# Attention of the next block beside a matmul stream: another order of its steps, of their loads, and of the sums for the second matmul

## What is computed

```python
scores = scale * np.matmul(q_c, k_full.transpose(0, 1, 3, 2))
scores = scores - np.max(scores, axis=-1, keepdims=True)
a = np.exp(scores)
a = a / (np.sum(a, axis=-1, keepdims=True) + 1e-09)
out[:, :, c_start:c_end] = np.matmul(a, v_full)
...
h = x @ w_in            # 3072 x 512 by 512 x 2048
g = h * np.cos(h)
x = g @ w_out           # by 2048 x 512
...
h = np.maximum(np.maximum(x @ w1, x @ w2), x @ w3)   # by 512 x 768 each
return h @ w_out        # by 768 x 512
```

## Time and profile before

| | |
|---|---|
| median of 3 runs | 1004.28 us (1001.45 to 1005.49) |
| the profiled execution's own time | 1003.52 us |
| its span in the trace | 1001.7 us |
| TensorE matmul busy | 962.1 us (96%) |
| VectorE / ScalarE / GpSimd busy | 675.9 (67%) / 516.0 (52%) / 210.2 us (21%) |
| mean granted TensorE clock | 0.983 |

### The profile page before, as it was taken

One profiled execution on the slowest core, in us unless ns is written; L12 is line 12 of the kernel. 1 busy time (PEld: TensorE's weight loads), 2 busy tenths in 40 slices (PEclk: granted clock), 3 DMA queues, 4 the chain that ended last, 5 costly groups with the idle time before them and its releaser, 6 DMA issues.

```text
span 1001.7 us, 18402 instructions
## 1 busy us (share of the span) xinstructions
PE 962.1 (96%) x7564; PEld 933.3 (93%) x7564; DVE 675.9 (67%) x926; ACT 516.0 (52%) x689; POOL 210.2 (21%) x231
## 2 busy tenths in 40 slices
PE   5989999999999999999999999999999999999998
PEld 4878889898989899989999999999999999999998
DVE  4355666566665568997998989866736546577761
ACT  1586786867778788333433334543323224444441
POOL 3341111112121212100100000662100000584610
PEclk6799999999999999999999999999999999999999
DMA  9983656574653434443445434432020031324532
GB/s 223 227 212 101 185 149 187 145 201 129 192 165 111 149 131 155 149 145 125 149 145 172 148 106 133 140 120 92 32 95 32 33 127 48 121 95 146 192 116 84
DMA packets 65395, 135.41 MB, mean 135 GB/s; under 512 B 5920, under 2 KB 27424, under 8 KB 65312
## 3 DMA queue, kind: packets, MB, share of 16 engines
q1 hardware_dynamic: 54944, 98.58, 34.2%
q0 software_dynamic: 10368, 35.66, 10.8%
HBM read 87.03 MB, written 47.19 MB: 134 GB/s over the span
## 4 chain that ended last, share of the span: by engine, by line
PE 73%; ACT 10%; DVE 9%; DMA 4%; issue 3%; POOL 1%; SPq 1%; DVEq 0%; ACTq 0%
PE ps L595 23%; PE ps L597 22%; PE ps L596 22%; PE ps L611 2%; DVE work L1178 2%; ACT work L901 2%; PE ps L636 2%; DVE units L1215 2%; ACT work L896 1%; ACT work L903 1%; PE ps L645 1%; DMA early_qk<-qk_in 1%; DVE ssum L1145 1%; ACT work L893 1%; ACT work L872 1%
## 5 line engine op out<-in xcount | busy, mean ns | idle before, releaser
L595 PE MATMUL ps<-units 128*128 128x384 f32 (+1 forms) x1940 | 611.1, 315 | 8.3 <-DVE units L1215 2.0
L597 PE MATMUL ps<-units 128*128 128x384 f32 (+1 forms) x1940 | 602.9, 311 | 0.0
L596 PE MATMUL ps<-units 128*128 128x384 f32 (+1 forms) x1940 | 602.6, 311 | 0.0
L595 PEld LDWEIGHTS ps<-units 128*128 128x128 f32 x1940 | 369.4, 190 | 20.2 <-issue 6.9
L596 PEld LDWEIGHTS ps<-units 128*128 128x128 f32 x1940 | 369.6, 191 | 0.0
L597 PEld LDWEIGHTS ps<-units 128*128 128x128 f32 x1940 | 369.2, 190 | 0.0
L921 ACT CAST units<-work 128x1024 fp32r<-128x1024 f32 x96 | 85.7, 939 | 123.9 <-DVE work L1201 106.6
L1076 ACT COPY work<-ps 128x384 f32<-128x384 f32 (+1 forms) x144 | 63.6, 454 | 146.9 <-PE ps L597 146.8
L1173 DVE SCALAR_TENSOR_TENSOR work<-work 128x768 f32<-128x768 f32 x64 | 62.2, 972 | 71.8 <-ACT work L896 71.8
L1215 DVE TENSOR_TENSOR units<-work,units 128x1024 fp32r<-128x1024 f32 x96 | 102.1, 1105 | 12.2 <-ACT units L921 12.2
L486 POOL DMA_DIRECT2D g_dram<-work x64 | 46.8, 731 | 291.4 <-DVE work L1178 286.7
(11 more groups left out here) (96 smaller groups left out, 845.4 us busy)
## 6 DMA issues: line engine op xcount, KB each, us to landing
g_dram<-work POOLq DMA_DIRECT2D x64, 384.0 KB, 3.3
work<-g_dram SPq DMA_DIRECT2D x48, 512.0 KB, 3.7
work<-qk_in SPq DMA_DIRECT2D x36, 384.0 KB, 5.3
work<-v_in SPq DMA_DIRECT2D x40, 256.0 KB, 5.0
work<-w_in POOLq DMA_DIRECT2D x40, 256.0 KB, 3.6
h_dram<-work SPq DMA_DIRECT2D x24, 384.0 KB, 2.9
work<-h_dram SPq DMA_DIRECT2D x18, 512.0 KB, 3.9
work<-y_dram SPq DMA_DIRECT2D x8, 768.0 KB, 6.5
```

Of the source, the lines that this page charges most:

```text
L595: pe.matmul(o, wh, mh, start=start, stop=False, skip_group_check=onto)
L596: pe.matmul(o, wh, ml, start=False, stop=False, skip_group_check=onto)
L597: return pe.matmul(o, wl, mh, start=False, stop=stop, skip_group_check=onto)
```

## The change

- **Opening:** on TensorE the second `turn_probs` now comes ahead of the third `scores_of`; raw w_in is loaded behind all values of block 0, and its casts (`high_wi(0)` to `(3)`) come behind the last `x_high`.
- **Block 0** (`attend0`): the scores of subs 3 to 5 move from beside f = 0, 2, 4 to f = 2, 5, 8, the exponentials from f = 5 to f = 9, the transposes of the probabilities to f = 10, 11, 12, the values to f = 12, 13, 14, the transposes of the output to f = 13, 14, 15. The scores of subs 6 to 8, which stood here, move to block 1.
- **Block 1** (`attend1`): has what block 0 had before, the scores of its own three subs among it, and those of block 2 at f = 8, 11, 14.
- **Blocks 2 to 6** (`attend`): the first `turn_out` moves from f = 4 to f = 5; `values(n + 1)` comes right ahead of `scores_of` at f = 6 (was f = 7), `values(n + 2)` likewise at f = 9 (was 11); the last `turn_out` at f = 11. VectorE's `x_low(n)` moves from f = 4 to f = 6, behind a `normalise` and a `shift`.
- **Loads:** values have three buffers for three blocks in place of two, and SyncE's list alternates values and scores' operands in the new order; g's first load comes before the last values.
- **Weight and g sums:** `sums_w1(5)` and `sums_g(0)` are made in block 6, the other g sums of block 7 come earlier, `sums_w1(6)` moves from f = 14 to f = 10, `sums_w1(7)` from the unit stage (behind unit 2) to f = 14 of block 7, with a buffer of its own; `low_w1(6)` and `low_w1(7)` stand together ahead of `sums_g(3)`. `load_w1(6)` stays where it was; `load_w1(7)` is issued right behind it, once it has landed.
- **y stage:** two more buffers let `y_sum(blk, 2)` and `(blk, 3)` be made ahead, before the block begins; they lie in the buffer of `load_v2(0)`, which therefore waits for the end of y's last block load (`y_ready` = 28) and not for `w2_ready` = 9 as before.

```diff
+        def y_extra(blk, i):
+            at = 9984 + 768 * (i - 3)
+            return work[:, at:at + 768].rearrange("p (k t) -> p k t", k=2) if blk and i > 2 else raw_y[:, 4, :, :]
+
+        def source_y(blk, p):
+            if p in (5, 6, 4):
+                return y_extra(blk, {5: 2, 6: 3, 4: 4}[p])
+            return raw_y[:, {1: 0, 7: 1, 2: 2, 3: 3}[p], :, :]
...
@@ -327,8 +338,9 @@
                     sp.wait_ge(g_stored[i % 3], 16 * (i // 3) + 16)
                 if n >= 2:
                     sp.wait_ge(g_ready, n - 1)
+                elif n == 1:
+                    sp.wait_ge(pv_done, SUBS)
                 else:
-                    sp.wait_ge(pv_done, SUBS)
                     sp.wait_ge(qk_done, SUBS)
...
@@ -393,30 +405,41 @@
             load_qk(0)
             load_qk(1)
             load_v(0)
-            load_wi(0)
             load_qk(2)
             load_v(1)
             load_v(2)
-            for f in range(1, 6):
+            for f in range(4):
                 load_wi(f)
             for n in range(NSUB, 2 * NSUB):
                 load_qk(n)
-                load_wi(2 * n)
-                load_wi(2 * n + 1)
+                load_wi(2 * n - 2)
+                load_wi(2 * n - 1)
             for n in range(NSUB, 2 * NSUB):
                 load_v(n)
-                if n < 2 * NSUB - 1:
-                    load_wi(2 * n + 6)
-                    load_wi(2 * n + 7)
+                load_wi(2 * n + 4)
+                load_wi(2 * n + 5)
             for n in range(2 * NSUB, 3 * NSUB):
                 load_qk(n)
-            load_v(2 * NSUB)
+                load_v(n)
             load_qk(3 * NSUB)
-            for n in range(2 * NSUB + 1, SUBS):
-                load_v(n)
+            load_qk(3 * NSUB + 1)
+            load_v(3 * NSUB)
+            load_qk(3 * NSUB + 2)
+            load_qk(3 * NSUB + 3)
+            for n in range(3 * NSUB, SUBS, NSUB):
+                if n + 3 == SUBS:
+                    load_g(0)
+                load_v(n + 1)
+                load_v(n + 2)
                 if n + 3 < SUBS:
-                    load_qk(n + 3)
-            for n in range(4):
+                    if n + 4 < SUBS:
+                        load_qk(n + 4)
+                    load_v(n + 3)
+                    if n + 5 < SUBS:
+                        load_qk(n + 5)
+                    if n + 6 < SUBS:
+                        load_qk(n + 6)
+            for n in range(1, 4):
...
             def load_w1(p):
-                if p:
+                if p == FPAIRS - 1:
+                    pool.wait_ge(o_ready, SUBS)
+                elif p:
...
             def load_v2(v):
-                if v == 0:
-                    pool.wait_ge(w2_ready, UNITS)
-                else:
-                    pool.wait_ge(y_ready, 7 * NBLK2)
+                pool.wait_ge(y_ready, 7 * NBLK2)
...
@@ -561,7 +583,8 @@
                     load_w1(5)
                 if t == 7 and p == 3:
                     load_w1(6)
-            load_w1(7)
+                    pool.wait_ge(w1_landed, 32 * 7)
+                    load_w1(7)
             load_w2(0)
...
-            def attend_first(f):
+            def attend0(f):
                 n = NSUB
+                if f == 2:
+                    scores_of(n)
+                elif f == 5:
+                    scores_of(n + 1)
+                elif f == 8:
+                    scores_of(n + 2)
+                elif f == 10:
+                    turn_probs(n)
+                elif f == 11:
+                    turn_probs(n + 1)
+                elif f == 12:
+                    turn_probs(n + 2)
+                    values(n)
+                elif f == 13:
+                    turn_out(n)
+                    values(n + 1)
+                elif f == 14:
+                    turn_out(n + 1)
+                    values(n + 2)
+                elif f == 15:
+                    turn_out(n + 2)
...
                     turn_probs(n + 1)
+                elif f == 5:
                     turn_out(n)
                 elif f == 6:
                     turn_probs(n + 2)
+                    values(n + 1)
                     if later:
                         scores_of(n + NSUB)
-                elif f == 7:
-                    values(n + 1)
                 elif f == 8:
                     turn_out(n + 1)
-                elif f == 9 and later:
-                    scores_of(n + NSUB + 1)
+                elif f == 9:
+                    values(n + 2)
+                    if later:
+                        scores_of(n + NSUB + 1)
                 elif f == 11:
-                    values(n + 2)
-                elif f == 12:
                     turn_out(n + 2)
-                    if later:
-                        scores_of(n + NSUB + 2)
+                elif f == 12 and later:
+                    scores_of(n + NSUB + 2)
 
...
+            def beside0(f, i):
+                n = NSUB
+                if f + 4 < NF:
+                    high_wi(f + 4)
+                if f == 9:
+                    exps(0, NSUB, n + NSUB)
+                elif f == 11:
+                    copy_probs(n)
+                elif f == 15:
+                    x_high(n + 2)
+                if f % 2:
+                    evacuate(i)
+                    if f == 11:
+                        copy_probs(n + 1)
+                    elif f == 13:
+                        x_high(n)
+                    if i:
+                        cosine(i - 1)
+                if f == 12:
+                    copy_probs(n + 2)
+                elif f == 14:
+                    x_high(n + 1)
...
+            def beside_last(f, i):
+                if f % 2:
+                    evacuate(i)
+                    cosine(i - 1)
+                if f == 1:
+                    high_w1(5)
+                elif f == 4:
+                    high_g(0, 0)
+                    high_g(0, 1)
+                elif f == 8:
+                    high_g(1, 0)
+                    high_g(1, 1)
+                elif f == 12:
+                    high_g(2, 0)
+                    high_g(2, 1)
+
...
-                if i == 2:
-                    dve.wait_ge(y_ready, 7 * blk + 2)
-                if i == 3:
-                    dve.wait_ge(y_ready, 7 * blk + 4)
-                o, in0, in1 = ((e, b12, b11), (b12, b22, b12), (e, b22, e), (e, b21, e))[i]
+                b11, b12, b21, b22 = [raw_y[:, q, :, :] for q in range(4)]
+                e = [y_extra(blk, j) for j in (2, 3, 4)]
+                if not blk and i >= 2:
+                    dve.wait_ge(y_ready, 2 * i - 2)
+                elif blk and i == 2:
...
+            def beside(t, f, i):
+                n = NSUB * (t + 1)
+                if f == 3:
+                    normalise(n)
+                elif f == 9:
+                    normalise(n + 2)
+                if f % 2:
+                    pair(i)
+                if f == 2:
+                    sums(0, NSUB, NSUB + t + 1)
+                elif f == 5:
+                    sums_w1(t - 1)
+                elif f == 6:
+                    normalise(n + 1)
+                    if t < NBLK - 2:
+                        shift(n + NSUB)
...
+            def beside_last(f, i):
+                if f % 2:
+                    pair(i)
+                if f == 0:
+                    sums_g(1)
+                elif f == 2:
+                    low_w1(5)
+                elif f == 4:
+                    low_g(0, 0)
+                    low_g(0, 1)
+                elif f == 6:
+                    sums_g(2)
+                elif f == 8:
+                    low_g(1, 0)
+                    low_g(1, 1)
+                elif f == 10:
+                    sums_w1(6)
+                elif f == 12:
+                    low_g(2, 0)
+                    low_g(2, 1)
+                elif f == 14:
+                    sums_w1(7)
+
...
                     y_low(blk + 1, 5)
-                    y_sum(blk + 1, 2)
+                    y_low(blk + 1, 2)
                 if n < UNITS_ALL:
                     c12(n)
                 if n and before < UNITS_A and before % NB2:
                     c21(before)
                 if renew:
-                    y_low(blk + 1, 2)
                     y_low(blk + 1, 6)
                     y_low(blk + 1, 3)
                 if renewed:
                     y_low(blk, 7)
-                    y_sum(blk, 3)
                     y_low(blk, 4)
+                if n < UNITS_A and u == UNITS - 2 and blk < NBLK2 - 1:
+                    y_sum(blk + 1, 2)
+                    y_sum(blk + 1, 3)
                 if n < UNITS_A and u == UNITS - 3 and blk < NBLK2 - 1:
                     y_sum(blk + 1, 0)
                     y_sum(blk + 1, 1)
```

317 lines of the change are left out of this document (159 added, 158 removed).

## The result

The changed kernel takes 1018.63 us (median of 4 runs, 1014.81 to 1024.56), the kernel before 1004.88: a ratio of 1.0147, 95% interval 1.0115 to 1.0179. It is slower by some 14 us. 5 were forecast, and the time lies outside the stated range. The profiled execution has a span of 1015.5 us, against 1001.7.

The account below looks back on a forecast made before the run. TensorE's matmuls, busy 96% of the span, were taken to bound the kernel. Terms +5.8 + 0 - 7.3 + 4.0 + 2.5 = +5.0 on the profiled 1003.5 gave 1008.5 us, range 995 to 1015.

Parts of the forecast that it names:

- Blocks 2 to 6, -7.3 forecast: Blocks 2 to 6: five 1.59 us waits of the first turn_out for normalise go; -7.3, bounds -7.9 and -4.8.
- counted from the durations it ends 0.6 ahead of the second `turn_out`: Blocks 2 to 6: x_low(n), in its new place behind normalise(n + 1) and a shift, is still 0.6 us early.
- Block 0: Block 0: evacuate(3) waits for tile 0's store, 9.0 us to land, delaying exponentials and x_low; block 1 starts at 90.3, +5.8.
- Rival 2: Block 0: tile 0's store lands as fast as the median one, 5.0 us less, 1003.5; chance 0.15.
- The opening: Start of the kernel: block 0 begins some 0.8 us earlier, at 32.0, counted inside block 0's sum.
- Block 1: Block 1: takes over block 0's old work; first turn_out waits 2.4 us against 2.6 before; 0, bounds -1.5 and +2.
- Unit stage: +4.0 forecast: Block 7 and unit stage: TensorE's waits total 8 us against 4.0 before; +4.0, bounds -4.0 and +6.
- VectorE's stand: Block 7: VectorE stands still 6.0 us ahead of sums_w1(6), waiting for its load behind a store on GpSimd.
- still cost: Unit stage: the results' sums at the border of the first eight units cost 1.3 us as before.
- y stage: +2.5 forecast: y stage: load_v2(0) waits for y_ready = 28, three v2 sets follow one another; +2.5, bounds 0 and +5.5.
- The rival for the case "slower": y stage: v2 sets cost 5.5 not 2.5 us, plus 1.5 for half clocks in block 0; 1013, chance 0.15.
- new waits in blocks 2 to 6 for `x_low`: Blocks 2 to 6: a listed sign that the prediction is wrong; no size given.

Follow-up runs that it names:

- e3_w1load: Changed kernel with load_w1(1) to load_w1(5) issued behind the store of tile 8t + 5, not 8t + 6, on GpSimd: 1005.88 us, ratio 1.0007.
- a1_xlow: Changed kernel with VectorE's x_low(n) ahead of normalise(n + 1) and the shift in blocks 2 to 6, weight sums behind them: 1006.8 us, ratio 1.0029.
- a3_xlow_qk: Changed kernel with both the edits of a1_xlow and a2_qk: 1002.3 us, ratio 0.9995 to the kernel before.
- a2_qk: Changed kernel with SyncE loading the scores' operands of sub n + 5 ahead of the values of sub n + 3: 1018.13 us, ratio 1.0148.
- e1_w17_old: d2_all with weight set 7 as in the kernel before (load behind last store, sums_w1(7) at unit 2, low_w1(7) at unit 4): 992.55 us, ratio 0.9868.
- e2_w17_mid: d2_all keeping the early load of set 7, but sums_w1(7) ahead of unit 2's g sums and low_w1(7) ahead of unit 3's: 992.5 us, ratio 0.9874.
- b1_yback: Changed kernel with the y stage as before: no buffers for sums ahead, load_v2(0) behind w2_ready = 9: 1015.63 us, ratio 1.0116.
- e4_mid_w1load: e2_w17_mid with the edit of e3_w1load: 992.11 us, ratio 0.987 to the kernel before.
- d2_all: d1_block0_old with b1_yback's edit, sums_w1(6) back at f = 14, load_w1(7) behind tile 61's store, sums_w1(7) behind the last gated: 992.92 us, ratio 0.9889.
- d1_block0_old: a3_xlow_qk with blocks 0 and 1 in the order of before but the changed opening: 995.13 us, ratio 0.9889.

## Why the prediction was wrong

- **Blocks 2 to 6, -7.3 forecast, +8.3 measured. The step that failed** is "counted from the durations it ends 0.6 ahead of the second `turn_out`". It ended 1.8 to 2.5 us behind. The durations were right; the start of the chain was not. The count took `evacuate` to come with TensorE's step, as it does in the trace of before (197.28 and 197.42). But it is held there by a landing store, which came just then, and the landing does not get earlier with TensorE. In block 3 of the changed kernel `evacuate` is 2.5 us behind the step; without this `x_low` would have ended some 0.7 ahead of the second `turn_out` (an estimate: 2.5 less the wait of 1.83). e3_w1load shows the cause, a1_xlow and a3_xlow_qk that the list could have absorbed it. A second omission: the order of SyncE's list, where a load of values stands ahead of the third scores' load (4.3 us of waits). By a2_qk that is worth little alone, and by a3_xlow_qk against a1_xlow 3 to 5 us (1006.8 to 1002.3, by the ratios 3.4) once the other is mended. A third is the granted clock, 0.96 in blocks 5 and 6, which the term put at nothing. The prediction's bound of -4.8 allowed 0.5 us for each late `x_low`, a quarter of what came.
- **The gain itself was right**: with the list and the loads mended, blocks 2 to 6 give 7.0.
- **Block 0: right in its chain.** The store of tile 0 was issued at 46.27, and the evacuate that waited for it began 9.5 us later (9.0 forecast), after 4.85 us of ScalarE's idle time (5 forecast); block 0 took 58.3 us, as worked out (90.3 - 32.0). Rival 2, the fast landing, fell. The opening was mis-sized: it ended 3.3 us earlier than forecast (28.7 and not 32.0), and at 28.5 to 29.7 in the other traces that have it. Part of its gain of 4.1 is luck of the first trace of before: its second trace ends the opening at 30.5, and against that the gain is 1.8.
- **Block 1: right** (0 forecast). With the three groups of scores that moved in, 3.2 us, it took 48.9 where 49.8 was forecast; its first `turn_out` waited 1.7 and not 2.4.
- **Unit stage: +4.0 forecast, -0.3 measured.** VectorE's stand was right (6.0 and 5.78), and so was `low_g(3)`: it ended at 422.7, 5.8 us later in its stage than before (5.7 forecast). TensorE waited 4.3 (5.9 forecast), 3.9 of it in unit 0 for `evacuate` and next to nothing for `low_g(3)`. But the 1.3 us that "still cost" at the border were gone, and units 8 to 16 took 40.3 us in place of 44.7: 2.0 of waits, and 2.3 of matmul time, since the granted clock there was 0.96 before and 1.00 now. That VectorE has no backlog there because the weight sums are already made fits e1_w17_old and e2_w17_mid, where `sums_w1(7)` stands at unit 2 again and both waits are back. The forecast added new waits to old ones which the same edit removed.
- **y stage: +2.5 forecast, +4.3 measured**, of which 3.2 are the v2 chain (2.8 with b1_yback), -1.5 the earlier y sums, and 2.7 what the trace of before lacked by chance. The terms of its sum (0.6, 1.0, 1.8, less 0.7) make 2.7, not 2.5, the waits in the prediction's first paragraph make 19.7 and not 16, and the second rival's price is 5.0 in the list of rivals and "some 4" in the text; none of these slips matters to the outcome.
- **Rivals and chances.** The rival for the case "slower" was named for the v2 chain and the clock, while 8.3 of the 13.8 came from blocks 2 to 6, for which no rival was written down, though "new waits in blocks 2 to 6 for `x_low`" stood among the signs of being wrong, and came. The term on which 7 us hung had a margin of 0.6 us, and a margin that thin should have been a rival of its own. Losing the gain alone makes the sum 1015.8, and the +8.3 that came makes it 1024.1; the range ended at 1015. That the median of 1018.63 lies below the second is no merit of the forecast: the stage up to block 1 and the unit stage were each 4.3 us better than forecast.

**What beats both kernels.** e4_mid_w1load, e2_w17_mid, e1_w17_old and d2_all all take 992 to 993 us, 1.1 to 1.3% under the kernel before, and d1_block0_old 995; all keep the opening, the new order of blocks 2 to 6 and its loads, and the early g sums. The step that counts for most is the old order of blocks 0 and 1 on top of a3_xlow_qk (d1_block0_old); what the four do beyond it is not clear of noise.

## What to carry to other kernels

When an edit takes a wait from the busiest engine, what followed that engine closely may be held by something else that came at nearly the same time and stays where it was. List such places (here an `evacuate` that started 0.14 us behind TensorE's step and was released by a landing store) and follow each one forward to the next thing that TensorE wants. Here a load issued right ahead of a store on the same queue was part of that store's landing time (5.7 and 3.9 us). Where a gain of some us rests on a counted margin under 1 us, count it from the latest of all starts, and give the other outcome its own price.

## What was not expected of the hardware

- A store of 384 KB issued 3.3 us behind a load of 512 KB (two of 256 KB) from GpSimd released its `evacuate` 5.7 us after its issue, and 3.9 us when the load was issued 9.4 us ahead of it; the DMA share meanwhile was 0.69 and 0.79. The Trainium skill, "DMA: Bandwidth & Descriptors", section "Two DMAs through the same engine are not ordered", says that within one queue of one engine descriptors start in order; by that the store stands behind the load, and these two landings agree. For the store of tile 0, the taking turns between queues of the same page's section "Queues, rings and completion order" did not make the landing short (9.5 us under a DMA share of 1.03).
- The opening is not the same in each execution of one kernel: block 0 began at 32.80 in one trace of the kernel before and at 30.46 in the other. Over the first 28.5 us the granted clock was 0.65 in the first trace of before, 0.76 in the second, and 0.82 in that of the changed kernel.
- A wait of TensorE can have a second price in the clock. In blocks 2 to 6 the granted clock was 1.00 in every block of before, a3_xlow_qk and e3_w1load, and 0.96 in two of the five blocks of the changed kernel (with `x_low` waits of 2.06 and 2.46 in them) and in three of a2_qk. Not every such wait had it: block 2 of the changed kernel, with one of 2.51, shows 1.00.
